# Rows of the cosine and sine tables, of their copies and of the ring 378 columns apart instead of 384

## The reference

```
x: (4, 3008, 256)
X = fft(x, axis=1); X = fft(X, axis=2); x = X.real        # 12032 tokens of 256
h = x @ w_in;  r = max(h, 0);   x = (r * r) @ w_out        # first layer, d_ff 2048
h = x @ w_in2; g = h * cos(h);  out = g @ w_out2           # second layer, d_ff 2048
```

## Time and profile before

| | us |
|---|---|
| median of 3 runs | 1969.04 |
| lowest, highest of them | 1968.5, 1969.79 |
| the profiled execution | 1968.96 |
| its span, first to last instruction | 1967.0 |
| PE busy in it | 1957.6 |
| DVE busy | 1431.9 |
| ACT busy | 1260.8 |

### The profile page before, as it was taken

One profiled execution on the slowest core, in us unless ns is written; L12 is line 12 of the kernel. 1 busy time (PEld: TensorE's weight loads), 2 busy tenths in 40 slices (PEclk: granted clock), 3 DMA queues, 4 the chain that ended last, 5 costly groups with the idle time before them and its releaser, 6 DMA issues.

```text
span 1967.0 us, 21365 instructions
## 1 busy us (share of the span) xinstructions
PE 1957.6 (100%) x8463; PEld 1615.2 (82%) x8463; DVE 1431.9 (73%) x1669; ACT 1260.8 (64%) x1323; POOL 0.2 (0%) x4
## 2 busy tenths in 40 slices
PE   8999999999999999999999999999999999999999
PEld 6888888888888888888888888888888888888887
DVE  8978767776876876776777687676677667667665
ACT  7867656755765765665675576566566567567555
POOL 0000000000000000000000000000000000000000
PEclk9999999999999999999999999999999999999999
DMA  7641111113013111100011311200000000000000
GB/s 286 228 148 66 62 67 64 38 46 130 33 51 103 50 61 67 53 6 22 32 38 35 109 54 51 91 30 6 11 22 6 11 22 6 0 22 1 0 11 21
DMA packets 37811, 106.30 MB, mean 54 GB/s; under 512 B 4296, under 2 KB 14664, under 8 KB 37456
## 3 DMA queue, kind: packets, MB, share of 16 engines
q1 hardware_dynamic: 35696, 90.79, 13.6%
q10 hardware_dynamic: 2016, 14.16, 2.1%
HBM read 86.39 MB, written 27.97 MB: 58 GB/s over the span
## 4 chain that ended last, share of the span: by engine, by line
PE 96%; DMA 1%; DVE 1%; ACT 1%; SPq 0%; issue 0%; DVEq 0%; ACTq 0%
PE ps L1003 96%; DMA stage_t<-tables 1%; DMA stage_a<-w2i 1%; ACT tab_even L560 0%; DVE gh L918 0%; DVE kbuf L955 0%; DVE u L960 0%; DVE weo L753 0%; DVE u L961 0%; PE ps L1165 0%; SPq L376 0%; DVE gh L915 0%; DVE wo L826 0%; DVE est L816 0%; DVE wsp_last L747 0%
## 5 line engine op out<-in xcount | busy, mean ns | idle before, releaser
L1003 PE MATMUL ps<-gh,wo 128*128 128x502 f32 x4596 | 1132.9, 396 | 1.1 <-DVE gh L918 0.8
L1003 PEld LDWEIGHTS ps<-gh,wo 128*128 128x128 f32 x4596 | 881.0, 192 | 191.5 <-DVE gh L918 2.4
L1003 PE MATMUL ps<-y,wi 128*128 128x502 f32 x2304 | 568.4, 396 | 0.0
L1003 PEld LDWEIGHTS ps<-y,wi 128*128 128x128 f32 x2304 | 441.8, 192 | 93.0
L968 DVE TENSOR_TENSOR u<-kbuf,ps 128x1004 f32<-128x1004 int32 x192 | 230.3, 1199 | 366.9 <-ACT kbuf L728 366.9
L918 DVE TENSOR_TENSOR gh<-u,gh 128x1004 fp32r<-128x1004 f32 x383 | 458.8, 1198 | 3.7 <-ACT gh L638 2.2
L728 ACT ACTIVATE kbuf<-ps 128x1004 int32<-128x1004 f32 x192 | 193.9, 1010 | 369.6 <-PE ps L1003 369.6
L713 ACT ACTIVATE u<-u 128x1004 f32<-128x1004 f32 x192 | 200.8, 1046 | 175.0 <-DVE u L961 174.7
L1003 PE MATMUL ps<-eo,weo 128*128 128x502 f32 x1146 | 297.7, 395 | 0.0
L1003 PEld LDWEIGHTS ps<-eo,weo 128*128 128x128 f32 x1146 | 219.6, 192 | 47.1
L740 ACT ACTIVATE u<-u 128x1004 f32<-128x1004 f32 x192 | 200.5, 1044 | 65.2 <-DVE u L968 65.2
(11 more groups left out here) (107 smaller groups left out, 339.1 us busy)
## 6 DMA issues: line engine op xcount, KB each, us to landing
ring<-scratch_t SPq DMA_DIRECT2D x72, 384.0 KB, 4.0
xin<-x SPq DMA_DIRECT2D x36, 512.0 KB, 3.3
out<-io SPq DMA_DIRECT2D x23, 502.0 KB, 3.3
scratch_t<-tables ACTq DMA_DIRECT2D x12, 768.0 KB, 4.6
io<-scratch_eo SPq DMA_DIRECT2D x11, 502.0 KB, 4.7
scratch_eo<-est SPq DMA_DIRECT2D x14, 376.5 KB
stage_t<-tables SPq DMA_DIRECT2D x6, 768.0 KB, 16.3
tab_odd<-scratch_t ACTq DMA_DIRECT2D x2, 2304.0 KB, 12.0
```

The source lines that it names most:

```text
L1003: op = pe.matmul(out_, a, b, start=start and i == 0, stop=stop and i == len(todo) - 1)
```

## The change

One number: `KS` becomes `KH`, 378. The rows then stand directly behind each other. Nothing else in the code differs, and the values that are computed are the same.

```diff
 KT = 3
 KH = 378
 
-KS = 384
+KS = KH
 KP = H // 2 + 1
```

## The result

The changed kernel takes 1892.8 us (median of 4 runs, 1892.54 to 1893.19); the kernel before takes 1969.19 beside it. The ratio is 0.9612, with a 95% interval of 0.9596 to 0.9629: 3.9% faster, 76 us. The forecast was 1968.8, no change; it is 76 us off and the time lies far outside the range of 1967.0 to 1972.5. What happened is the rival that I had priced and given 6 in 100: the pace of the long matmuls.

What follows compares the result with a forecast made beforehand. TensorE's own pace was taken to bound the kernel. From 1968.96 us, 0.03 for the even table's load and 0.18 for the odd table's were taken off, zero added for reads: 1968.8 us, range 1967.0 to 1972.5.

Steps and rivals of the forecast that it cites:

- What bounds the kernel: Whole kernel: TensorE busy 1957.6 of 1967.0 us; all else together has 9.4 us of its idle time to win.
- TensorE's reads: 324 matmuls of 378 columns on ring and tables: zero change taken, 3.2 us kept for the range.
- The 10 ns: Largest pace difference among 502-column matmuls, 223.3 against 233.3 ns; used as price for 324 matmuls on moved rows, 3.2 us.
- rival B: Long 502-column matmuls' pace shifts; a gain of over 0.2%, anywhere between 1895 and 1965 us, had chance 0.06.
- Head, conversions, copies: Even table's load 0.03 us less, conversions zero with 0.8 us kept for DVE's, copies and odd table 0.18 us less.
- The 0.2 us gain: Odd table's loads beside those of `stage_a`: 74 KB fewer, at most 0.2 us of it reaching the end.
- The ring's slots: 72 ring transfers lose 1.56% of bytes, gain hidden; 1.2 us spare at the closest place, so no change.
- the fifth more that I allowed for: Ring loads from odd starts up to a fifth slower, 0.8 us on a landing of 4.0, within the spare time.
- Rivals A and D: A: 324 matmuls read moved rows more slowly, large case 0.10; D: ring slots land late, over 0.2% slower, 0.02.
- 0.80 on no change: Whole kernel: chance given to a measured time within 0.2%, 3.9 us, of the forecast.

Runs made afterwards that it cites:

- short64: Kernel before, rows 384 apart, plus one 64-column matmul in mix step 2 of tile 0 and up step 2 of every later tile: 1893.98 us, ratio 0.9617.
- ring alone: Kernel before with only the ring's rows in SBUF 378 apart, tables and device memory at 384: 1901.64 us, ratio 0.9657.
- stops: Kernel before, all rows 384 apart, with TensorE made to stand still in up step 8 of tiles 5 and 9: 1944.76 us, ratio 0.9876.
- odd table alone: Kernel before with only the odd table's rows in SBUF 378 apart, even table, ring and device memory at 384: 1892.07 us, ratio 0.9608.

## Why the prediction was wrong

**What bounds the kernel: right.** TensorE full from 90 us to the end, "only its own pace counts". Nothing else took part in the result.

**TensorE's reads: the term of zero was right, and its frame was wrong.** The nine ring matmuls take 1.56 to 1.58 us where I counted 1.56. The step that failed is that I priced the 324 matmuls whose rows move as if they were the only ones whose pace the change could touch, and put the pace of all others at no change. They are 4% of the matmuls. What they do to the others, by the pace in which they leave TensorE, is 7700 x 10 ns, 77 us. One argument for the zero was weak all the same: the rows of `lastc` start at multiples of 16 bytes, so they are no example of the 8-byte starts of the moved rows, as I had it.

**The 10 ns: read, used as a price, not pursued.** The earlier trace rows show two paces for one shape at one clock. I wrote that nothing in the profile shows the cause, put it into rival B and gave a gain by it 0.06, because "the place of the shift is steady, and the change touches neither those operands nor the order". Both halves are true, and the conclusion is wrong. A steady place means that it is bound to something in the program, and the place was to be had: the last 24 matmuls at the fast pace stand ahead of the `lastc` group, and in the trace of before the 233 ns begin right behind it, at 109 us, a group that reads exactly the rows that are moved. As the earlier trace rows end with the `lastc` group, it took one more row of the view to see it. Read so, the change touched the one point at which the kernel before falls slow, and the question would have been whether it still falls; half and half would have been a fair chance. The price itself was right: "the 7429 matmuls after 240 us hold 74 us", 1895 as the end of B's span, 1892.8 measured.

**Head, conversions, copies: right, and without weight.** ACT's conversions take 1456 ns (1462 before), DVE's 925 (926). The first piece is taken at 18.95 us instead of 18.26, where I had 0.03 us earlier; in the other kernels of this study with that wait it lay between 18.4 and 18.9, whatever their rows. The 0.2 us gain isn't seen: the long piece of the chain starts 0.3 us later.

**The ring's slots: right.** TensorE stood idle 0.0 us ahead of them; landings take 3.9 us at the median (4.0 before), so the fifth more that I allowed for isn't seen.

**Rivals A and D: wrong.** By the starts of the groups no matmul on moved rows takes over 3 ns longer, and no slot came late.

**The chances.** 0.80 on no change was too much with an unexplained 4% in the rows, whose trigger I hadn't looked for.

What is still open: why TensorE has these two paces. At 233 ns a weight load takes 192 ns at the mean and at 223 ns 188 (PEld busy 1615.2 us in all before, 1582.7 after), and the load is issued about as a matmul starts in both. The runs show what tips the pace (length of a matmul, distance of rows, a stop, most likely a late weight load beside one of the four), but not the rule by which a given disturbance ends in the one or the other. Why `lastc` with rows 384 apart ends in the slow pace and `fb` doesn't, and why rows 378 apart turn this round while 380, 382 or 384 columns keep the fast pace in both, isn't settled either.

## What to carry to other kernels

Where a tight row of equal matmuls has more than one pace at one granted clock, find the first matmul at the slower pace and what stands directly ahead of it, before any edit is priced: the price of an edit there is that of all matmuls behind it. Divide starts, not durations, and do it for several stretches of the program. If TensorE is the bound, one short matmul, another column count or a row distance that isn't 384 is worth a try at the point of the fall, and a gain or loss of some per cent after a harmless edit may be this and not the edit. All of this rests on one kernel.

## What the runs showed of the hardware that I had not expected

- TensorE issues matmuls of 502 columns with 128 x 128 fp32r operands back to back at 223.3 or at 233.3 ns, at granted clock 1.00 of the 2.4 GHz level, and holds either for over a thousand microseconds. The matmuls of 378 columns between them keep about 173 to 176 ns in both.
- 64 columns ahead of a long row tip 233 to 223 ns (four of four, in two kernels: at 160 and 810 us of the kernel before with short matmuls, at 158.5 and 934.6 of short64), 256 tip 223 to 233 ns (four of four, in two kernels), 128 and 192 leave 223 ns alone (each four of four).
- A stop of TensorE of 2.5 us brings 223 ns back (three of three). Behind the two stops of one kernel the granted clock was 0.91 over 20 us, behind the one of the other it stayed 1.00.
- The fast pace fell by itself in four kernels (ring alone, stops, odd table alone, short64), each time with a weight load that waited for DVE beside the same one of four matmuls. The times of the first two spread over 5 and 9 us, those of the changed kernel, of short64 and of rows 382 apart over less than 1.
